# Products of ones between the thirds of w1's products and behind both spreadings of G

## The reference, cut to what matters

```python
def _moe2_ref(x, w_gate, w1, w2):          # x (3072, 384), w1 (8, 384, 1024), w2 (8, 1024, 384)
    logits = x @ w_gate
    expert_idx = np.argmax(logits, axis=1)
    ...                                     # gate_w: the softmax probability of the chosen expert
    for e in range(E):
        mask = expert_idx == e
        if not mask.any():
            continue
        h = np.maximum(x[mask] @ w1[e], 0.0)
        out[mask] = gate_w[mask, None] * (h @ w2[e])
```

## Time and profile before

| | us |
|---|---|
| median of 3 runs | 278.39 |
| lowest, highest | 277.00, 281.28 |
| the profiled execution | 277.07 |
| its span, first to last instruction | 275.20 |
| TensorE busy in it | 258.7 |
| mean granted TensorE clock in it | 0.985 |

### The profile page before, as it was taken

One profiled execution on the slowest core, in us unless ns is written; L12 is line 12 of the kernel. 1 busy time (PEld: TensorE's weight loads), 2 busy tenths in 40 slices (PEclk: granted clock), 3 DMA queues, 4 the chain that ended last, 5 costly groups with the idle time before them and its releaser, 6 DMA issues.

```text
span 275.2 us, 10447 instructions
## 1 busy us (share of the span) xinstructions
PE 258.7 (94%) x4505; PEld 218.1 (79%) x4505; DVE 154.7 (56%) x320; ACT 89.3 (32%) x175; POOL 30.5 (11%) x45
## 2 busy tenths in 40 slices
PE   8789899999999998999998799999999999999992
PEld 8768687888787884433477599999999999999991
DVE  5787798889898874435032594532523534435313
ACT  1224445545545543031230552222222222222200
POOL 3222122222212215000000000000000000000000
PEclk9999999999999999999999779999999999999999
DMA  5975899999999999999507500030110300300203
GB/s 155 340 241 171 290 319 387 392 390 378 403 403 407 330 416 417 424 355 427 230 2 265 197 0 0 0 115 0 53 61 0 114 0 0 114 0 16 101 0 120
DMA packets 16324, 55.30 MB, mean 201 GB/s; under 512 B 1936, under 2 KB 5200, under 8 KB 15408
## 3 DMA queue, kind: packets, MB, share of 16 engines
q1 hardware_dynamic: 13216, 43.90, 43.1%
q10 hardware_dynamic: 3088, 11.14, 10.5%
HBM read 50.32 MB, written 4.72 MB: 200 GB/s over the span
## 4 chain that ended last, share of the span: by engine, by line
PE 86%; DMA 4%; DVE 3%; issue 2%; SPq 1%; ACT 1%; POOL 0%; ACTq 0%; DVEq 0%; POOLq 0%
PE ps L1189 12%; PE ps L1188 12%; PE ps L1190 12%; PE ps L922 8%; PE ps L945 6%; PE ps L960 6%; PE ps L969 5%; PE ps L934 4%; PE ps L1173 4%; PE ps L1060 4%; PE ps L1082 4%; PE ps L974 3%; DMA ind<-dmaj 2%; DMA wraw<-wb 2%; PE ps L1029 2%
## 5 line engine op out<-in xcount | busy, mean ns | idle before, releaser
L823 DVE SCALAR_TENSOR_TENSOR hl<-ps,hh 128x512 fp32r<-128x512 f32 x48 | 33.0, 690 | 58.7 <-ACT hh L568 58.7
L1189 PE MATMUL ps<-w2l,hh 128*128 128x384 f32 x192 | 65.3, 340 | 0.0
L1188 PE MATMUL ps<-w2h,hh 128*128 128x384 f32 x192 | 65.1, 339 | 0.0
L1190 PE MATMUL ps<-w2h,hl 128*128 128x384 f32 x192 | 65.0, 338 | 0.0
L568 ACT ACTIVATE hh<-ps 128x512 fp32r<-128x512 f32 x48 | 28.7, 600 | 75.8 <-PE ps L1173 75.8
L1189 PEld LDWEIGHTS ps<-w2l,hh 128*128 128x128 f32 x192 | 36.6, 191 | 1.7
L1188 PEld LDWEIGHTS ps<-w2h,hh 128*128 128x128 f32 x192 | 36.6, 191 | 0.7
L1190 PEld LDWEIGHTS ps<-w2h,hl 128*128 128x128 f32 x192 | 36.6, 191 | 0.0
L435 POOL TENSOR_TENSOR kt<-intk,kttab 128x384 f32<-128x384 f32 x24 | 24.2, 1009 | 71.0 <-DVE rkb L638 62.8
L638 DVE TENSOR_TENSOR rkb<-ind,tab 128x1024 f32<-128x1024 f32 x24 | 29.9, 1247 | 1.4 <-DMA ind<-dmaj 1.4
L922 PE MATMUL ps<-rkb 64*64 64x128 f32 x768 | 27.3, 273 | 0.0
(11 more groups left out here) (163 smaller groups left out, 295.9 us busy)
## 6 DMA issues: line engine op xcount, KB each, us to landing
ind<-dmaj SPq DMA_DIRECT2D x22, 512.0 KB, 8.1
wearly<-wa ACTq DMA_DIRECT2D x21, 512.0 KB, 7.1
intk<-tmaj SPq DMA_DIRECT2D x24, 384.0 KB, 6.9
wearly<-wa SPq DMA_DIRECT2D x4, 1536.0 KB, 11.3
out<-acc SPq DMA_DIRECT2D x5, 768.0 KB, 3.6
wlate<-wa SPq DMA_DIRECT2D x4, 768.0 KB, 9.3
wlate<-wa SPq DMA_DIRECT2D x2, 1536.0 KB, 11.5
wmid<-wa SPq DMA_DIRECT2D x1, 1536.0 KB, 8.4
```

Of the source, the lines that this page charges most:

```text
L823: v.scalar_tensor_tensor(out=hl[:, f % 4, :], in0=ps[:, f % 4, :], scalar=0.0, in1=hh[:, f % 4, :].bitcast(F32), op0=ALU.max, op1=ALU.subt ...
L1188: mm(o, a_h, w2h[:, f, :], start=(f == 0), stop=False)
L1189: mm(o, a_h, w2l[:, f, :], start=False, stop=False)
L1190: ins = mm(o, a_l, w2h[:, f, :], start=False, stop=(f == KF - 1))
```

## The change

Three calls are added, all for the first expert only. Between the thirds of G's products two products of ones into bank 0 go before the waits of q = 1 and q = 2; behind `g_spread(0)` two into bank 2; behind `g_spread(1)` three into bank 3. That is 2 + 2 + 2 + 3 = 9 products of 128 columns, without a semaphore.

```diff
                 for q in range(KD):
+                    if first and q:
+                        warm(2, 0)
                     pe.wait_ge(w1b_in[q], k * 16 + 16)
...
                 g_spread(0)
+                if first:
+                    warm(2, 2)
...
                 h1(0, 2, True)
                 pe.wait_ge(gst_ready[1], k + 1)
                 g_spread(1)
+                if first:
+                    warm(3, 3)
                 pe.wait_ge(gst_ready[3], k + 1)
                 h1(0, 1, True)
                 h1(0, 3, True)
```

## The result

The first measurement gave 281.15 us as the median of 4 executions (279.78 to 282.86) beside 279.27 for the kernel before (277.00 to 281.28), a ratio of 1.0126 with a 95% interval of 1.008 to 1.0171. Two repetitions of the same comparison gave 278.80 us in 12 executions (ratio 1.0043, 1.0006 to 1.0080) and 279.45 in 12 (0.9987, 0.9913 to 1.0060). The kernel before against itself gave 1.0032 (0.9995 to 1.0070). So the 1.3% of the first four executions is not borne out. Over all of them the changed kernel stands at 279.4 us (28 executions, mean 279.39 with a standard error of 0.37), the kernel before at 279.0 (157 executions, 278.93 with 0.13). I had forecast 276.1, in a range of 274.5 to 279.0; both the 281.15 and the 279.4 lie above it. The gain of 2.3 us did not come, and the executions of either kernel scatter over some 8 us.

A forecast was written before the change was run, and what follows sets the result against it. TensorE was taken to set the time, with a low clock from 154.4 to about 161.2. Keeping it up saves 0.46 + 1.76 + 0.06 = 2.28 us at no added cost: 278.39 - 2.28 = 276.1 us, range 274.5 to 279.0.

The forecast's parts named there:

- What bounds the kernel: Whole kernel: TensorE, busy 258.7 of 275.2 us, sets the time; its clock is low for about 6.8 us from 154.4.
- The sum of 2.28 us: From 156.27 to 161.42: gain if the clock stays up, 0.46 + 1.76 + 0.06 us.
- my first two terms: Start of the dense stretch: two h products gain 0.46 us, the twelve products of h2(0, 0) gain 1.76.
- Behind the spreadings: 0: After both spreadings of G: ones hide in waits for gst, cost 0; bounds 0 to 0.47 and 0 to 0.35 us.
- my bound of 0.35 us behind the second spreading: Behind the second spreading at 1.2 GHz: six passes of ones end some 0.35 us past 156.27.
- Between the thirds: 0: Between the thirds of w1's products: ones hide in the wait for the last third's transfer, cost 0.
- the other bound in the text, 0.94 us: Between the thirds: cost of all of 0.94 us if the last third had landed with the second.
- Against the median: 278.39 - 2.28 = 276.1: Whole kernel: the 2.28 us gain taken from the median of 278.39 gives the predicted 276.1 us.
- The rows against each other: Windows 10 to 14 and 102 to 106 held the clock at 2.49 and 2.89 busy of 4; 150 to 154 would reach 3.2.
- Rival 1: Clock falls at the same place; ones do not count, or not enough: 278.4 to 278.8 us, chance 0.17.
- Rival 2: Fall put off to the start of the dense stretch, down 6.8 us: net +1.1, 279.5 us, chance 0.12.
- The page of the Trainium skill: Holes before the fall: it warns only of clearly longer gaps, so by it ones there give 278.4 us, no gain.

The follow-up runs named there:

- thirds-only kernel: Kernel before plus only the 2 + 2 products of ones between the thirds of w1's products, none behind the spreadings: 279.99 us.
- bare: Kernel before without products of ones among and behind the gate products: 280.55 us without the change, 278.79 us with it.
- denser stretch: Kernel before with two ones after the first gate product, 12 instead of 8 among, 4 instead of 6 behind: mean 278.56 us without the change, 276.94 with.

## Why the prediction was wrong, point by point

- **What bounds the kernel.** Right: TensorE, and the clock's low level in it costs some 0.4 us for each microsecond of low time (0.37 over the executions of before).
- **The sum of 2.28 us.** Right in size. Where the clock held, 2.10 us were gained up to the h product behind h2(0, 0), for the 2.22 of my first two terms. VectorE and ScalarE held nothing back: behind 161.29 of the changed kernel the dense loop ran as reckoned.
- **Behind the spreadings: 0.** Right at the high clock: 4.18 us with and without. The wait for VectorE's copy of gst stayed the last one (0.26 us of it left). With the clock down my bound of 0.35 us behind the second spreading was too small: 0.53 in the one profile that shows it.
- **Between the thirds: 0.** Wrong. I had the other bound in the text, 0.94 us for landed data at the high clock, with the wait for the transfer as cover. But a call costs 0.71 us and not 0.47, so two cost 1.42. Where the clock held, some 0.4 us of that lay on the path. With the clock fallen in the gate stretch TensorE takes 8.5 to 10.2 us from its second gate product to G's first, instead of 6.0; the transfers are issued near the start of that stretch and don't wait for it, so the cover is gone, and the term is 1.73 us, measured.
- **"Against the median: 278.39 - 2.28 = 276.1."** This is the step that failed, together with the term before. I made the sum against one profile, took its fall at 154.4 for a property of the kernel, and subtracted what it costs from the median of all executions. In nine profiles of kernels with the old gate stretch the clock fell there five times (144.9, 145.0, 146.6, 148.1, 148.5), once at 154.4, and three times not at all in the second mixture. Where it falls ahead of the change, it is back by 153.4 to 155.3 anyway, before the dense stretch, and of that fall there is nothing left to save; in one of the five it fell again at 160.2.
- **The rows against each other.** I read the thin stretches of the earlier trace rows and left out the gate stretch, since its busy time is full. The five falls there came after TensorE had been busy without a break for 1.3 to 3.2 us, behind a hole of 0.44. The busy time of the rows doesn't tell whether the clock holds.
- **The rivals.** None of them was it. Rival 1 came out at no gain as well, but for another reason, that products of ones don't count; they do, as the pairs on the bare and on the denser stretch show. Rival 2 was seen in one execution of the thirds-only kernel. A fall before the change, with the products then on the path, was missing.
- **The net of zero.** Sorted by low time: under 7 us lie 8 of 28 executions of the changed kernel and 17 of 157 of before, so the change does save some falls. But in that class their means are 277.3 against 276.7 us, from 7 to 11 us of low time 279.4 against 278.0, above 11 us 281.1 against 279.8; the three differences have standard errors of 0.5, 0.4 and 0.4. At like low time the changed kernel is 0.5 to 1.4 us slower, which fits products that lie on the path (0.4 us where the clock held, 1.73 where it had fallen). Against that stand 1.4 us less of mean low time, worth some 0.5 us. That the two cancel is read from these means and not from a run that separates them; the 0.4 and the 1.73 us each come from one or two profiles.
- **The page of the Trainium skill.** The Trainium skill's advice in "TensorE: Matmul & The Clock Gate", "Why this matters for your kernels", on idle gaps, which I set against my forecast, does not explain the outcome. By it filling holes shorter than the gaps it warns of should change nothing. The runs don't bear this out: the longest hole just ahead of the fall was 1.12 us in the earlier trace rows and 0.44 us for the five in the gate stretch. The 1.88 to 2.78 us ahead of the three falls on the denser stretch are nearer to such gaps and say less against it. On the denser stretch the change took the low time from 7.9 to 2.8 us and the mean from 278.6 to 276.9.

## What to carry to other kernels

One profile shows where the clock fell once; before a sum is built on it, look at the mean clock of many executions and at two or three more traces. Products that keep TensorE at work are free only in a wait that stands even when TensorE comes late, so place them in the hole where the trace shows the longest wait and not in front of work that may be ready, and read from several traces when the data land. And fill the thin stretches in their order: no gain could be measured behind a stretch that often lost the clock, and 1.6 us, with a standard error of 0.5, behind one that held it.

## What the runs showed of the hardware

- The same program loses the clock at places that differ from one execution to the next. Low time went from 1.1 to 19.6 us, and the time from 274.2 to 282.7 us, over the executions of the kernel before.
- The clock can fall in a stretch in which TensorE is busy throughout: 24 products of 8 columns with 8 products of 128 columns among them, after 1.3 to 3.2 us without a break, with one hole of 0.44 us ahead of it.
- The landing of w1's last third moves too. Its transfer took from 4.9 to 7.4 us from issue to landing, and TensorE waited from nothing to 2.78 us for it.
